# Expert limits searched by base-32 digits of a whole number, and batch folds spread over the items

## The chip, the cores and the metric

The kernel runs on one core of a Trainium2 chip. The metric is the device time of one execution in microseconds (us), the median of several. TensorE (PE in the rows; PEld is its weight load), VectorE (DVE), ScalarE (ACT) and GpSimd (POOL) each run their own list of instructions and wait for each other by semaphores. SyncE (SP) issues most transfers.

## The reference

A two-dimensional Fourier transform (real part) is followed by two mixtures of experts. What the change touches is the transform and the first routing:

```python
X = np.fft.fft(np.fft.fft(x, axis=1), axis=2).real       # x: 4 x 2496 x 256
logits = x @ w_gate                                        # N = 9984 tokens, E = 8 experts
order = np.argsort(-logits.flatten())
for idx in order:                                          # greedy, highest logit first
    tok, e = idx // E, idx % E
    if assigned[tok] >= 0 or counts[e] >= cap: continue    # cap = N // E = 1248
    assigned[tok] = e; counts[e] += 1
...
h = np.maximum(x[mask] @ w1[e], 0.0); out[mask] = h @ w2[e]
# then a second mixture, by argmax, with gates
```

## The kernel before

**First stage: the transform along the sequence.** The list `work_list` has 18 items (batch, part, half). TensorE runs 20 matmuls for an item into two banks; ScalarE copies one bank out (`half`), VectorE joins it with the other (`joined(n)`, two or three instructions of lines 1201 to 1212, which also bump `s_seq`). TensorE may start item n when `joined(n - 3)` is done. Items 0 to 3 are batch 0, items 4 to 7 batch 1, items 8 to 11 batch 2, items 12 and 13 the middle column of all batches, items 14 to 17 batch 3. The input of each batch comes in two transfers and is first folded: `fold(n)` on VectorE (lines 1182 and 1185) makes `even`, a pair on GpSimd (lines 553 and 559) makes `odd`, and ScalarE's `edges(n)` picks two columns. Folds 0 and 1 are batch 0, folds 2 and 3 batch 1, and so on. The table `FOLDS_AT` says after which item's join VectorE issues which fold, and ScalarE the matching `edges`.

**Second stage: features.** 40 tiles, two matmuls each; VectorE copies the odd ones out, ScalarE the even ones, SP stores them.

**Third stage: the search for limits.** Seven phases (`ph`), each closing one expert. In a phase, `name8` finds each token's best open expert (`best`, a one-hot `hot8`), 78 columns of 128 tokens. Then four rounds of `search`: VectorE compares each token's `best` with 32 probes (`above`, four pieces by `CHUNKS`), TensorE counts them per expert with 78 small matmuls whose weights are `above[:, j, :]` (`above_count`), VectorE sets `passes`, one matmul turns them into a step, and VectorE moves the lower bound (`floor`, `move`) and makes the next 32 probes. After the fourth round it marks the tokens above the limit (`new_b`, `ind8`), TensorE counts them (`new_count`, line 819) and then runs `gate_rows` (line 799, 32 matmuls for later use) while VectorE updates the counts and names again. So in each phase but the first, round 0's matmuls stand behind `gate_rows` in TensorE's queue.

**After it** come the slots (one-hot matmuls, from about 369 us) and the two mixtures, from about 412 us to the end.

Of the kernel before, what the change touches and what calls it, by code (L numbers as in the profile page):

```python
# [18 lines left out]
F32 = mybir.dt.float32  # L19
F32R = mybir.dt.float32r  # L20
BF16 = mybir.dt.bfloat16
I32 = mybir.dt.int32
# [6 lines left out]
P = 128  # L29
B, S, D = 4, 2496, 256  # L30
N = B * S
# [23 lines left out]
HOTS = 4  # L55
PROBES = 32
ROUNDS = 4
CHUNKS = (0, 24, 48, 68, N // P)
DCH = D // P
FCH = F // P  # L60

# [17 lines left out]
def turns(gi):  # L79
# [8 lines left out]
_W = [("feat_c", XC), ("feat_s", XC), ("featT_c", 2 * P), ("featT_s", 2 * P), ("ident", P), ("tri", P),  # L88
      ("iota", P), ("prefer", E), ("base1", E), ("base2", E),
      ("sign", 1), ("lane", 1), ("lane2", 1), ("valid", TPE), ("beyond", TPE), ("span", G2 + 1),  # L90
      ("part_lane", NT1), ("fresh4", E * (1 + GT)), ("fresh2", E * 3), ("parts", PROBES * ROUNDS)]
COL = {}
_at = 0
for _n, _w in _W:
# [5 lines left out]
def constants():  # L100

    n = 2 * np.arange(NC * P)[None, :] + np.arange(2)[:, None]
    ang = 2 * np.pi * ((n[:, :, None] * np.arange(KH)) % S) / S
    keep = (n <= HALF)[:, :, None]
    edge = np.where((n == 0) | (n == HALF), 0.5, 1.0)[:, :, None]
    lay = lambda t: np.ascontiguousarray(
        t.reshape(2, NC, P, KH).transpose(2, 0, 1, 3)).astype(np.float32)
    cos_n, sin_n = lay(np.cos(ang) * keep * edge), lay(np.sin(ang) * keep)
    c = np.zeros((P, NCONST), np.float32)

    def put(name, v):
        a, b = COL[name]
        c[:, a:b] = v

    d = np.arange(P)[:, None]
    l = np.arange(XC)[None, :]
    put("feat_c", np.cos(2 * np.pi * ((d * l) % D) / D))
    fs = -np.sin(2 * np.pi * ((d * l) % D) / D)
    fs[0] = (-1.0) ** np.arange(XC)
    put("feat_s", fs)  # L120
    put("featT_c", np.concatenate([c[:, slice(*COL["feat_c"])][:, h * P:(h + 1) * P].T for h in range(2)], 1))
    put("featT_s", np.concatenate([c[:, slice(*COL["feat_s"])][:, h * P:(h + 1) * P].T for h in range(2)], 1))
    put("ident", np.eye(P))
    put("tri", np.arange(P)[:, None] < np.arange(P)[None, :])
    put("iota", np.arange(P)[None, :])
    put("prefer", (E - np.arange(E))[None, :])
    put("base1", (np.arange(E) * TPE * P)[None, :])
    put("base2", (np.arange(E) * REG)[None, :])
    put("span", (np.arange(G2 + 1) * W2)[None, :])
    put("fresh4", (np.arange(E * (1 + GT)) % (1 + GT) != 0)[None, :])  # L130
    put("fresh2", (np.arange(E * 3) % 3 != 0)[None, :])
    p = np.arange(P)[:, None]
    put("sign", np.where(np.arange(P) == 0, 1.0, -1.0)[:, None])
    put("lane", p)
    parts = (np.arange(PROBES) + 1) * float(PROBES) ** -(np.arange(ROUNDS)[:, None] + 1)
    put("parts", parts.reshape(1, -1))
    put("lane2", p + P)
    put("part_lane", p / (np.arange(NT1) + 1.0)[None, :])
    put("valid", (np.arange(TPE) * P + p < CAP))
    put("beyond", 16.0 * E * REG * (np.arange(TPE) * P + p >= CAP))  # L140
    return cos_n, sin_n, c


class Count:
# [5 lines left out]
    def link(self, ins):  # L150

        ins.then_inc(self.sem, 1)
        self.n = self.n + 1
        self.eng.wait_ge(self.sem, self.n)


def build_program(nc, x, x_rev, cos_n, sin_n, const, wg1, w1a, w2a, w2a_t, wg2, wo2, w1b, w2b, out):
    ctx = ExitStack()
    with ctx, nc.allow_non_contiguous_dma("a few rows of logits"):
        def sb(name, shape, dt=F32):  # L160
            return ctx.enter_context(nc.sbuf_tensor(name, shape, dt))
# [88 lines left out]
        def cc(name):  # L250
            return cst[:, COL[name][0]:COL[name][1]]
# [18 lines left out]
        ones_f = sb("ones_f", [1, P])  # L270
        taken = sb("taken", [P, T1])
        first_b = sb("first_b", [P, T1], BF16)
        floor, width = (sb(n, [P, 1]) for n in ("floor", "width"))
        at = 4 * WS + WE + 2 * FCH * GT * P


        def small(w):
            nonlocal at
            at += w
            return arena[:, at - w:at]  # L280

        steps = small(PROBES * ROUNDS)
        probe0 = small(PROBES)
        probe = [small(PROBES) for _ in range(2)]
        at = 4 * WS + WE
        open_log = small(E * NT1).rearrange("p (j e) -> p j e", e=E)
        slow_log = small(E * NT1)
        above = small(NT1 * PROBES // 2).bitcast(BF16).rearrange("p (j k) -> p j k", k=PROBES)
        hot8, ind8 = (small(NT1 * E // 2).bitcast(BF16).rearrange("p (j e) -> p j e", e=E) for _ in range(2))
        hot_b, ind = (small(W8 // 2).bitcast(BF16) for _ in range(2))  # L290
        assert at <= s0
        step_b = sb("step_b", [P, ROUNDS, P], BF16)
        passes = sb("passes", [PROBES, E], BF16)
        new_b = sb("new_b", [P, T1], BF16)
        floors = [sb(f"floor{u}", [P, 1]) for u in range(2)]
        move, top_i = sb("move", [P, 1]), sb("top_i", [P, 1], I32)
        surs = sb("surs", [P, E])
        gone = sb("gone", [P, T1])
# [108 lines left out]
        work_list = [(b, q, h) for b in range(3) for q in range(2) for h in range(2)]  # L407
        work_list += [(0, 2, h) for h in range(2)] + [(3, q, h) for q in range(2) for h in range(2)]
        MID_DONE = 4 * 3 + 2
        FOLDS_AT = {1: (2, 3), 2: (4,), 3: (5,), 4: (6,), 5: (7,)}  # L410
        SEQ_DONE = [4, 8, 12, NU]
        LAST_AT = 5
        assert LAST_AT % 2 and NB % 2
# [303 lines left out]
        def _(pe):  # L717
# [85 lines left out]
            def above_count(n):  # L803

                for c in range(len(CHUNKS) - 1):
                    pe.wait_ge(s_above, n * (len(CHUNKS) - 1) + c + 1)
                    for j in range(CHUNKS[c], CHUNKS[c + 1]):
                        mm = pe.matmul(bank[0][0:PROBES, 0:E], above[:, j, :], hot8[:, j, :],  # L808
                                       start=(j == 0), stop=(j == NT1 - 1))
                mm.then_inc(s_above_ps, 1)  # L810
                pe.wait_ge(s_pass, n + 1)
                pe.matmul(bank[1][:, 0:E], step_b[0:PROBES, n % ROUNDS, :], passes[:], start=True,
                          stop=True).then_inc(s_move_ps, 1)

            def new_count(ph, tokens):
# [332 lines left out]
        def _(dve):  # L1148
# [68 lines left out]
            for n in range(NU):  # L1217
# [5 lines left out]
                if n == NU - 3:  # L1223
                    feature_gates()

            for n in range(1, NB + 1, 2):
                feature_out(dve, dve.tensor_copy, n)

# [20 lines left out]
            dve.memset(zero_u[:], 0)  # L1249
            dve.memset(ones_f[:], 1.0)  # L1250
            dve.memset(ones8[:], 1.0)
            dve.memset(taken[:], FAR)
            dve.memset(gone[:], -FAR)
            dve.memset(left[:], float(CAP))
            dve.memset(first78[:], 1.0)
            link(dve.memset(left_open[:], float(CAP)))
# [1 line left out]
            dve.wait_ge(s_bound_ps, 1)  # L1258
            dve.tensor_reduce(top[0:1, :], bank[1][0:1, 0:P], AX.X, ALU.max).then_inc(s_bound, 1)
            dve.wait_ge(s_bound_ps, 2)  # L1260
            link(dve.tensor_copy(floor[:], bank[1][:, 0:1]))
            link(dve.tensor_scalar(top_i[:], floor[:].bitcast(I32), 0x7F800000, None, ALU.bitwise_and))
            dve.tensor_scalar(width[:], top_i[:].bitcast(F32), 4.0, None, ALU.mult)
            link(dve.tensor_scalar(floor[:], top_i[:].bitcast(F32), -2.0, None, ALU.mult))
            link(dve.tensor_scalar(steps, cc("parts"), width[:], None, ALU.mult))
            link(dve.tensor_scalar(probe0, steps[:, 0:PROBES], floor[:], None, ALU.add))
            for r in range(ROUNDS):
                ins = dve.tensor_scalar(step_b[:, r, :], ones_b[:], width[:], float(PROBES) ** -(r + 1), ALU.mult, ALU.mult)
            link(ins)

            def name8(src):

                link(dve.tensor_reduce(best[:, 0:NT1], src, AX.X, ALU.max))
                link(dve.tensor_tensor(best[:, 0:NT1], best[:, 0:NT1], taken[:, 0:NT1], ALU.min))
                link(dve.tensor_tensor(hot8[:], src, each_e(best), ALU.is_equal))

            def search(ph, r):

                n = ph * ROUNDS + r
                at_ = probe[r % 2] if r else probe0  # L1280
                low, nxt = (floors[(r + u) % 2][:] if r + u else floor[:] for u in range(2))
                for j0, j1 in zip(CHUNKS, CHUNKS[1:]):
                    dve.tensor_tensor(above[:, j0:j1, :], best[:, j0:j1, None].to_broadcast([P, j1 - j0, PROBES]),  # L1283
                                      at_[:, None, :].to_broadcast([P, j1 - j0, PROBES]), ALU.is_ge).then_inc(s_above, 1)
                dve.wait_ge(s_above_ps, n + 1)
                dve.tensor_tensor(passes[:], bank[0][0:PROBES, 0:E], left_open[0:PROBES, :], ALU.is_ge).then_inc(s_pass, 1)
                dve.wait_ge(s_move_ps, n + 1)
                link(dve.tensor_reduce(move[:], bank[1][:, 0:E], AX.X, ALU.max))
                if r + 1 < ROUNDS:
                    dve.tensor_scalar(probe[(r + 1) % 2], steps[:, (r + 1) * PROBES:(r + 2) * PROBES], move[:], low,  # L1290
                                      ALU.add, ALU.add)
                link(dve.tensor_tensor(nxt, low, move[:], ALU.add))

            src = log8
            for ph in range(E - 1):
                name8(src)
                for r in range(ROUNDS):
                    search(ph, r)
                thr_v = floors[ROUNDS % 2][:]
                link(dve.tensor_scalar(new_b[:, 0:NT1], best[:, 0:NT1], thr_v, None, ALU.is_ge))  # L1300
                dve.wait_ge(s_given, ph + 1)
                dve.tensor_tensor(ind8[:], hot8[:], each_e(new_b), ALU.mult).then_inc(s_new, 1)  # L1302
                link(dve.copy_predicated(taken[:, 0:NT1], new_b[:, 0:NT1].bitcast(U16), gone[:, 0:NT1]))
# [437 lines left out]
```

## Time and profile before

| | |
|---|---|
| median of 3 runs | 1447.54 us (1446.55 to 1448.35) |
| profiled execution | 1448.4 us, span 1446.6 us |
| mean granted TensorE clock over the span | 0.899 |
| PE busy | 1291.4 us, 89% |
| DVE busy | 702.1 us, 49% |
| POOL busy | 551.7 us, 38% |
| ACT busy | 336.5 us, 23% |

The span is what lies between the first and the last instruction; the execution's own time has 1.8 us around it. The busy share is an average over stages with different limits, so the stages have to be read one by one.

### The profile page before, as it was taken

Reading aid. Unit: us, or ns where it says so; the run is one execution under the profiler, and the core shown is the slowest. Engines: PE = TensorE matmul, PEld = TensorE weight load, DVE = VectorE, ACT = ScalarE, POOL = GpSimd, SP = SyncE. Lnnn points to the kernel's source line nnn. Section 1 sums busy time; section 2 is a strip of 40 time slices with the busy share of each in tenths; the row PEclk is TensorE's granted clock in tenths of the full one; section 3 lists DMA queues with packets and bytes.
Section 4 is the critical chain, followed back from the end, with each engine's and each line's share of the span. In section 5 each row is a group of like instructions: output and inputs, shape, how many; then the busy total and the mean of one; then the engine's idle time right before and its main releaser. Section 6 shows DMA issues by size and latency. Waiting matters only on the chain.

```text
span 1446.6 us, 31150 instructions
## 1 busy us (share of the span) xinstructions
PE 1291.4 (89%) x10763; PEld 1194.7 (83%) x10764; DVE 702.1 (49%) x1991; ACT 336.5 (23%) x840; POOL 551.7 (38%) x556
## 2 busy tenths in 40 slices
PE   5899657666389999999999999699999999999996
PEld 4567557665179998999989998699999999999996
DVE  2723677776744445444554344634343443343332
ACT  0102100000523333333333233112222222222221
POOL 2800230000035656566564754331344142444411
PEclk9999755555579999999999999799999999999998
DMA  9604620101012221232222222131122222222110
GB/s 346 213 1 152 221 89 31 60 31 60 1 34 92 79 79 62 78 98 77 74 66 79 82 71 77 39 103 44 37 100 73 73 69 73 70 81 95 45 40 23
DMA packets 70726, 116.21 MB, mean 80 GB/s; under 512 B 7784, under 2 KB 50545, under 8 KB 70640
## 3 DMA queue, kind: packets, MB, share of 16 engines
q1 hardware_dynamic: 46864, 72.40, 14.9%
q0 software_dynamic: 11808, 31.03, 6.5%
q10 hardware_dynamic: 11968, 11.63, 2.9%
q8 instruction: 55, 0.90, 0.3%
q14 instruction: 31, 0.25, 0.1%
HBM read 81.87 MB, written 34.45 MB: 80 GB/s over the span
## 4 chain that ended last, share of the span: by engine, by line
PE 75%; DVE 8%; issue 2%; POOL 1%; ACT 1%; DMA 1%; POOLq 0%; DVEq 0%; ACTq 0%
PE bank L869 22%; PE bank L871 22%; PE bank L870 21%; DVE arena L1283 3%; PE bank L799 3%; PE bank L808 3%; PE bank L863 1%; PE bank L950 1%; ACT hot_q L1036 1%; POOL weights_low L575 1%; PE bank L849 1%; DVE hot_r L1448 1%; DVE arena L1290 0%; DVE hot_q L1449 0%; DVE arena L1302 0%
## 5 line engine op out<-in xcount | busy, mean ns | idle before, releaser
L869 PE MATMUL bank<-weights_high,hT_high 128*128 (+1 forms) x1328 | 387.1, 292 | 2.5 <-DVE hT_low L1676 2.5
L870 PE MATMUL bank<-weights_low,hT_high 128*128 (+1 forms) x1328 | 379.3, 286 | 0.0
L871 PE MATMUL bank<-weights_high,hT_low 128*128 (+1 forms) x1328 | 379.2, 286 | 0.0
L869 PE MATMUL bank<-xT_high,weights_high 128*128 128x256 f32 (+1 forms) x1072 | 334.6, 312 | 2.3 <-DVE xT_low L1664 1.3
L871 PE MATMUL bank<-xT_high,weights_low 128*128 128x256 f32 (+1 forms) x1072 | 332.0, 310 | 0.0
L870 PE MATMUL bank<-xT_low,weights_high 128*128 128x256 f32 (+1 forms) x1072 | 331.1, 309 | 0.0
L869 PEld LDWEIGHTS bank<-weights_high,hT_high 128*128 128x128 f32 x1328 | 251.2, 189 | 2.8 <-issue 2.8
L871 PEld LDWEIGHTS bank<-weights_high,hT_low 128*128 128x128 f32 x1328 | 251.5, 189 | 0.0
L870 PEld LDWEIGHTS bank<-weights_low,hT_high 128*128 128x128 f32 x1328 | 250.8, 189 | 0.0
L869 PEld LDWEIGHTS bank<-xT_high,weights_high 128*128 128x128 f32 x1072 | 204.4, 191 | 16.8 <-DVE hT_low L1495 3.2
L871 PEld LDWEIGHTS bank<-xT_high,weights_low 128*128 128x128 f32 x1072 | 203.3, 190 | 11.3
L870 PEld LDWEIGHTS bank<-xT_low,weights_high 128*128 128x128 f32 x1072 | 203.4, 190 | 10.0
L1495 DVE SCALAR_TENSOR_TENSOR hT_low<-bank,hT_high 128x512 fp32r<-128x512 f32 (+1 forms) x192 | 114.4, 599 | 174.9 <-ACT hT_high L1055 168.8
L680 POOL DMA_INDIRECT out_y<-arena,tokb x86 | 84.9, 987 | 289.1 <-DVE tokb L1691 277.0
L1117 ACT ACTIVATE hT_high<-bank 128x512 fp32r<-128x512 f32 x172 | 103.0, 599 | 384.1 <-PE bank L871 384.1
L1676 DVE SCALAR_TENSOR_TENSOR hT_low<-bank,hT_high 128x512 fp32r<-128x512 f32 x172 | 118.4, 691 | 149.4 <-ACT hT_high L1117 141.0
L621 POOL DMA_INDIRECT arena<-spectrum,idxe x80 | 78.5, 982 | 168.7 <-PE bank L863 154.5
L1055 ACT ACTIVATE hT_high<-bank 128x512 fp32r<-128x512 f32 (+1 forms) x192 | 101.4, 528 | 125.5 <-PE bank L871 124.7
L752 PE MATMUL bank<-arena 128*128 128x312 f32 (+3 forms) x360 | 99.5, 439 | 21.2 <-DMA arena<-in_cos 15.0
L1688 DVE TENSOR_SCALAR arena<-bank,gate_tok 128x256 f32<-128x256 f32 x86 | 41.6, 484 | 157.0 <-PE bank L871 118.1
L808 PE MATMUL bank<-arena 128*32 128x8 bf16 x2184 | 69.1, 168 | 47.0 <-DVE arena L1283 45.3
L752 PEld LDWEIGHTS bank<-arena 128*128 128x128 f32 (+1 forms) x360 | 66.0, 185 | 53.3 <-issue 31.0
(232 smaller groups left out, 1446.7 us busy)
## 6 DMA issues: line engine op xcount, KB each, us to landing
arena<-middle ACTq DMA_DIRECT2D x44, 258.0 KB
spectrum<-arena SPq DMA_DIRECT2D x39, 256.0 KB, 2.2
arena<-in_w2a_t SPq DMA_DIRECT2D x8, 1024.0 KB, 5.1
raw<-in_w1a SPq DMA_DIRECT2D x8, 1024.0 KB
raw<-in_w2a SPq DMA_DIRECT2D x8, 1024.0 KB
raw<-in_w1b SPq DMA_DIRECT2D x8, 1024.0 KB
raw<-in_w2b SPq DMA_DIRECT2D x8, 1024.0 KB
arena<-in_x SPq DMA_DIRECT2D x4, 768.0 KB, 4.9
```

The source lines that it names most:

```text
L621: pool.indirect_dma_start(xg4[u], None, spectrum, bass.IndirectOffsetOnAxis(idxe[s][:, k:k + 1], 0)).then_inc(m1.got[u], 16)
L680: pool.indirect_dma_start(out, bass.IndirectOffsetOnAxis(tokb[j][:], 0), yb[j], None, bounds_check=N - 1, oob_is_err=False).then_inc(m2.se ...
L752: mm = pe.matmul(bank[2 * (n % 3) + r][0:m, 0:w], a, t[:, r, c, k0:k1], start=(c == 0), stop=(c == NC - 1))
L799: mm = pe.matmul(bank[3][:, f * LG:(f + 1) * LG], w2_t[:, c, f * P:(f + 1) * P], wgate2[:, c, :], start=(c == 0), stop=(c == DCH - 1))
L808: mm = pe.matmul(bank[0][0:PROBES, 0:E], above[:, j, :], hot8[:, j, :], start=(j == 0), stop=(j == NT1 - 1))
L869: pe.matmul(out_, a[0], b[0], start=start, stop=False)
L870: pe.matmul(out_, a[0], b[1], start=False, stop=False)
L871: return pe.matmul(out_, a[1], b[0], start=False, stop=stop)
L1055: act.activation(hT_split[0][:, f, 0:w], bank[2 + (gi * FCH + f) % 3][:, 0:w], ACT.Relu).then_inc(m1.h_high, 1)
L1117: act.activation(hT_split[0][:, q * FCH // HB:(q + 1) * FCH // HB, 0:W2], bank[H_BANKS[q]][:].rearrange("p (f n) -> p f n", n=W2), ACT.Rel ...
L1495: dve.scalar_tensor_tensor(out=hT_split[1][:, f, 0:w], in0=bank[2 + (gi * FCH + f) % 3][:, 0:w], scalar=0.0, in1=hT_split[0][:, f, 0:w].bi ...
L1676: dve.scalar_tensor_tensor(out=lo, in0=bank[H_BANKS[q]][:].rearrange("p (f n) -> p f n", n=W2), scalar=0.0, in1=hi.bitcast(F32), op0=ALU.m ...
```

## The change

Two edits. First, `FOLDS_AT` spreads folds 4 to 7 over items 3, 5, 7 and 9, where they stood after items 2, 3, 4 and 5. Second, the search works on whole numbers. `best` is scaled and rounded once a phase to a number of 20 bits (`digits[-1]`); the digits by shifts, four of 5 bits each; before each round one instruction subtracts the bound found so far and writes the result as bf16 (`key`). The 32 probes are always 1 to 32, stored once as a bf16 table `probes` of 32 x 78, made by one copy between the first two stages. The compare has the probe as its outer dimension and the column as its inner one, so TensorE's weights are now `above[:, :, j]`: 32 elements, 78 elements (156 bytes) apart, where they were 32 neighbours. Three pieces (12, 28 and 38 columns) stand where there were four (24, 24, 20 and 10).

```diff
-CHUNKS = (0, 24, 48, 68, N // P)
+CHUNKS = (0, 12, 40, N // P)
+BITS = PROBES.bit_length() - 1
+SHIFTS = [BITS * (ROUNDS - 1 - r) for r in range(ROUNDS)]
+LEVELS = 1 << BITS * ROUNDS
...
-        FOLDS_AT = {1: (2, 3), 2: (4,), 3: (5,), 4: (6,), 5: (7,)}
+        FOLDS_AT = {1: (2, 3), 3: (4,), 5: (5,), 7: (6,), 9: (7,)}
...
-                        mm = pe.matmul(bank[0][0:PROBES, 0:E], above[:, j, :], hot8[:, j, :],
+                        mm = pe.matmul(bank[0][0:PROBES, 0:E], above[:, :, j], hot8[:, j, :],
...
+            dve.wait_ge(s_seq, NU)
+            dve.wait_ge(s_half, NU)
+            dve.tensor_copy(probes, iota_b[:, 1:1 + PROBES, None].to_broadcast([P, PROBES, N // P]))
             for n in range(1, NB + 1, 2):
                 feature_out(dve, dve.tensor_copy, n)
...
-            for r in range(ROUNDS):
-                ins = dve.tensor_scalar(step_b[:, r, :], ones_b[:], width[:], float(PROBES) ** -(r + 1), ALU.mult, ALU.mult)
...
                 link(dve.tensor_reduce(best[:, 0:NT1], src, AX.X, ALU.max))
-                link(dve.tensor_tensor(best[:, 0:NT1], best[:, 0:NT1], taken[:, 0:NT1], ALU.min))
-                link(dve.tensor_tensor(hot8[:], src, each_e(best), ALU.is_equal))
+                dve.tensor_tensor(hot8[:], src, each_e(best), ALU.is_equal)
+
+            def whole():
+                link(dve.tensor_scalar(scaled, best[:, 0:NT1], scale[:].bitcast(F32), -0.5 * LEVELS, ALU.mult, ALU.max))
+                link(dve.scalar_tensor_tensor(out=digits[-1], in0=scaled, scalar=0.5 * LEVELS, in1=taken[:, 0:NT1],
+                                              op0=ALU.add, op1=ALU.min))
...
                 for j0, j1 in zip(CHUNKS, CHUNKS[1:]):
-                    dve.tensor_tensor(above[:, j0:j1, :], best[:, j0:j1, None].to_broadcast([P, j1 - j0, PROBES]),
-                                      at_[:, None, :].to_broadcast([P, j1 - j0, PROBES]), ALU.is_ge).then_inc(s_above, 1)
+                    dve.tensor_tensor(above[:, :, j0:j1], key[r % 2][:, None, j0:j1].to_broadcast([P, PROBES, j1 - j0]),
+                                      probes[:, :, j0:j1], ALU.is_ge).then_inc(s_above, 1)
+                if r == 0:
+                    for later in range(1, ROUNDS - 1):
+                        digit(later)
...
                 if r + 1 < ROUNDS:
-                    dve.tensor_scalar(probe[(r + 1) % 2], steps[:, (r + 1) * PROBES:(r + 2) * PROBES], move[:], low,
-                                      ALU.add, ALU.add)
-                link(dve.tensor_tensor(nxt, low, move[:], ALU.add))
+                    link(dve.tensor_scalar(key[(r + 1) % 2], digits[r + 1], move[:], low[r][:], ALU.subtract, ALU.subtract))
+                    dve.tensor_scalar(low[r + 1][:], low[r][:], move[:], float(PROBES) if r + 2 < ROUNDS else 1.0,
+                                      ALU.add, ALU.mult)
```

VectorE's order in the first stage, before, from the end of item 1's join on (lines 1182 and 1185 are a fold, 1201 with 1207 or 1210 a join):

```order
L1185 TENSOR_TENSOR arena<-arena 128x2x2x127
L1201 TENSOR_TENSOR arena<-arena,bank 128x313
L1207 SCALAR_TENSOR_TENSOR arena<-arena,bank 128x312
L1182 TENSOR_TENSOR arena<-arena 128x1536
L1185 TENSOR_TENSOR arena<-arena 128x2x3x127
L1201 TENSOR_TENSOR arena<-arena,bank 128x312
L1207 SCALAR_TENSOR_TENSOR arena<-arena,bank 128x311
L1182 TENSOR_TENSOR arena<-arena 128x1024
```

These are the end of fold 3, join 2, fold 4, join 3 and the start of fold 5. After, at the same place (the lines have moved by four):

```order
L1189 TENSOR_TENSOR arena<-arena 128x2x2x127
L1205 TENSOR_TENSOR arena<-arena,bank 128x313
L1211 SCALAR_TENSOR_TENSOR arena<-arena,bank 128x312
L1205 TENSOR_TENSOR arena<-arena,bank 128x312
L1211 SCALAR_TENSOR_TENSOR arena<-arena,bank 128x311
L1186 TENSOR_TENSOR arena<-arena 128x1536
L1189 TENSOR_TENSOR arena<-arena 128x2x3x127
L1205 TENSOR_TENSOR arena<-arena,bank 128x313
```

Join 3 now stands ahead of fold 4, and join 4 behind it. VectorE's order in the third stage, after, from the naming to round 1 of a phase:

```order
L1278 TENSOR_REDUCE best<-logits 128x78 [waits s_dve]
L1279 TENSOR_TENSOR arena<-logits,best 128x624 [waits s_dve]
L1283 TENSOR_SCALAR arena<-best,scale 128x78
L1284 SCALAR_TENSOR_TENSOR arena<-arena,taken 128x78 [waits s_dve]
L1289 TENSOR_SCALAR arena<-arena 128x78 [waits s_dve]
L1314 CAST arena<-arena 128x78 [waits s_dve]
L1295 TENSOR_TENSOR arena<-arena 128x32x12 [waits s_dve]
L1295 TENSOR_TENSOR arena<-arena 128x32x28
L1295 TENSOR_TENSOR arena<-arena 128x32x38
L1289 TENSOR_SCALAR arena<-arena 128x78 x2
L1301 TENSOR_TENSOR passes<-bank,left_open 32x8 [waits s_above_ps]
```

Lines 1283 to 1314 are four small instructions in a row ahead of the compares, where one small one (line 1274 of before) was.

## Rows read from the trace of the kernel before

**Rows 1.** The page: granted TensorE clock in 40 slices of the span.
```profile
PEclk9999755555579999999999999799999999999998
```
**Rows 2.** Windows by stage; columns: stretch, length, busy us of each engine, clock, DMA.
```profile
0.00:121.40 121.40, 100.23 (x369) 67.13 (x371) 46.52 (x65) 10.66 (x36) 42.46 (x23) 0.97 0.48 167
158.60:355.00 196.40, 126.92 (x2531) 118.80 (x2531) 154.43 (x344) 1.60 (x6) 32.50 (x25) 0.51 0.19 65
```
**Rows 3.** Timeline of TensorE, first stage: start, us, what, idle before.
```profile
54.67 44.74 PE L752 MATMUL bank<-arena 128*128 128x313 f32 x160 [6.20 <-DVE arena L1207]
```
**Rows 4.** Timeline of VectorE, first stage.
```profile
47.90 1.76 DVE L1182 TENSOR_TENSOR arena<-arena 128x1536 f32<-128x1536 f32 x1 [9.93 <-DMA arena<-in_x_rev]
49.70 4.05 DVE L1185 TENSOR_TENSOR arena<-arena 128x762 f32<-128x762 f32 x1
53.67 0.47 DVE L1201 TENSOR_TENSOR arena<-arena,bank 128x312 f32<-128x312 f32 x1
...
54.45 2.04 DVE L1182 TENSOR_TENSOR arena<-arena 128x1024 f32<-128x1024 f32 x1
56.52 2.71 DVE L1185 TENSOR_TENSOR arena<-arena 128x508 f32<-128x508 f32 x1
```
**Rows 5.** Timeline of ScalarE: the copy half way through item 8.
```profile
70.42 0.42 ACT L1018 COPY arena<-bank 128x313 f32<-128x313 f32 x1 [0.64 <-PE bank L752]
```
**Rows 6.** Windows as in rows 2: right after TensorE's stall; then its matmuls alone.
```profile
54.70:59.40 4.70, 4.70 (x9) 3.13 (x10) 4.67 (x3) 0.62 (x3) 4.45 (x3) 0.50 0.86 320
...
60.00:90.00 30.00, 30.00 (x115) 20.82 (x114) 1.00 0.33 114
```
**Rows 7.** Timeline of both engines, a last round of phase 4.
```profile
290.30 0.17 DVE L1288 TENSOR_REDUCE move<-bank 128x1 f32<-128x8 f32 x1 [0.28 <-PE bank L812]
290.90 2.96 DVE L1283 TENSOR_TENSOR arena<-best,arena 128x768 bf16<-128x768 f32 x4
291.91 2.57 PE L808 MATMUL bank<-arena 128*32 128x8 bf16 x78 [1.65 <-DVE arena L1283]
294.52 0.15 DVE L1286 TENSOR_TENSOR passes<-bank,left_open 32x8 bf16<-32x8 f32 x1 [0.65 <-PE bank L808]
295.15 0.16 DVE L1292 TENSOR_TENSOR floor<-floor,move 128x1 f32<-128x1 f32 x1
295.35 0.26 DVE L1300 TENSOR_SCALAR new_b<-best,floor 128x78 bf16<-128x78 f32 x1
```
**Rows 8.** Timeline of both engines, round 0 of phase 5.
```profile
297.04 6.99 PE L799 MATMUL bank<-wgate,arena 128*128 128x16 f32 x32
301.90 2.97 DVE L1283 TENSOR_TENSOR arena<-best,arena 128x768 bf16<-128x768 f32 x4
303.96 2.24 PE L808 MATMUL bank<-arena 128*32 128x8 bf16 x78
306.24 0.15 DVE L1286 TENSOR_TENSOR passes<-bank,left_open 32x8 bf16<-32x8 f32 x1 [1.37 <-PE bank L808]
```
**Rows 9.** VectorE's groups by form, 200 to 345 us: count, busy us, mean ns.
```profile
L1283 DVE TENSOR_TENSOR arena<-best,arena 128x768 bf16<-128x768 f32 x47 | 43.0, 954 | 0.8
L1283 DVE TENSOR_TENSOR arena<-best,arena 128x320 bf16<-128x320 f32 x24 | 11.6, 485 | 0.0
L1302 DVE TENSOR_TENSOR arena<-arena,new_b 128x624 bf16<-128x624 bf16 x5 | 4.0, 809 | 0.2
```
**Rows 10.** The same, 355 to 405 us.
```profile
L1328 DVE TENSOR_TENSOR arena<-arena 128x624 f32<-128x624 f32 x1 | 1.3, 1262 | 1.2 <-issue 1.2
...
L1432 DVE TENSOR_TENSOR arena<-arena 128x624 f32<-128x624 f32 x1 | 0.8, 808 | 0.0
...
L1434 DVE TENSOR_SCALAR pos_i<-pos 128x78 int32<-128x78 f32 x1 | 0.2, 202 | 0.0
```
**Rows 11.** Timeline of VectorE, rounds 2 and 3 of phase 0, beside GpSimd's weight splits.
```profile
176.22 5.92 DVE L1283 TENSOR_TENSOR arena<-best,arena 128x768 bf16<-128x768 f32 x4
...
182.67 0.15 DVE L1286 TENSOR_TENSOR passes<-bank,left_open 32x8 bf16<-32x8 f32 x1 [0.52 <-PE bank L808]
```

More of the change, by code:

```diff
@@ L90 @@
       ("sign", 1), ("lane", 1), ("lane2", 1), ("valid", TPE), ("beyond", TPE), ("span", G2 + 1),
-      ("part_lane", NT1), ("fresh4", E * (1 + GT)), ("fresh2", E * 3), ("parts", PROBES * ROUNDS)]
+      ("part_lane", NT1), ("fresh4", E * (1 + GT)), ("fresh2", E * 3)]
 COL = {}
@@ L134, in constants @@
     put("lane", p)
-    parts = (np.arange(PROBES) + 1) * float(PROBES) ** -(np.arange(ROUNDS)[:, None] + 1)
-    put("parts", parts.reshape(1, -1))
     put("lane2", p + P)
@@ L272, in build_program @@
         first_b = sb("first_b", [P, T1], BF16)
-        floor, width = (sb(n, [P, 1]) for n in ("floor", "width"))
+        bound, scale = sb("bound", [P, 1]), sb("scale", [P, 1], I32)
         at = 4 * WS + WE + 2 * FCH * GT * P
@@ L280, in small @@
             return arena[:, at - w:at]
-        steps = small(PROBES * ROUNDS)
-        probe0 = small(PROBES)
-        probe = [small(PROBES) for _ in range(2)]
+        digits = [small(NT1).bitcast(I32) for _ in range(ROUNDS)]
+        scaled = small(NT1)
+        key = [small(NT1 // 2).bitcast(BF16) for _ in range(2)]
         at = 4 * WS + WE
@@ L287, in build_program @@
         slow_log = small(E * NT1)
-        above = small(NT1 * PROBES // 2).bitcast(BF16).rearrange("p (j k) -> p j k", k=PROBES)
+        above = small(NT1 * PROBES // 2).bitcast(BF16).rearrange("p (k j) -> p k j", k=PROBES)
         hot8, ind8 = (small(NT1 * E // 2).bitcast(BF16).rearrange("p (j e) -> p j e", e=E) for _ in range(2))
@@ L291, in build_program @@
         assert at <= s0
-        step_b = sb("step_b", [P, ROUNDS, P], BF16)
+        at = gates_at + E * FCH * LG
+        probes = small(NT1 * PROBES // 2).bitcast(BF16).rearrange("p (k j) -> p k j", k=PROBES)
+        assert at <= arena_words
+        step_b = sb("step_b", [PROBES, 2, P], BF16)
         passes = sb("passes", [PROBES, E], BF16)
         new_b = sb("new_b", [P, T1], BF16)
-        floors = [sb(f"floor{u}", [P, 1]) for u in range(2)]
+        low = [sb(f"low{u}", [P, 1]) for u in range(ROUNDS)]
         move, top_i = sb("move", [P, 1]), sb("top_i", [P, 1], I32)
@@ L811, in above_count @@
                 pe.wait_ge(s_pass, n + 1)
-                pe.matmul(bank[1][:, 0:E], step_b[0:PROBES, n % ROUNDS, :], passes[:], start=True,
+                pe.matmul(bank[1][:, 0:E], step_b[:, n % ROUNDS == ROUNDS - 1, :], passes[:], start=True,
                           stop=True).then_inc(s_move_ps, 1)
@@ L1251, in _ @@
             dve.memset(ones8[:], 1.0)
-            dve.memset(taken[:], FAR)
-            dve.memset(gone[:], -FAR)
+            dve.memset(taken[:], float(2 * LEVELS))
+            dve.memset(gone[:], -1.0)
+            dve.memset(low[0][:], 0.0)
+            for u, v in enumerate((PROBES, 1)):
+                dve.memset(step_b[:, u, :], float(v))
             dve.memset(left[:], float(CAP))
@@ L1260, in _ @@
             dve.wait_ge(s_bound_ps, 2)
[L1261 to L1266, printed above, removed]
@@ L1267, in _ @@
-            for r in range(ROUNDS):
-                ins = dve.tensor_scalar(step_b[:, r, :], ones_b[:], width[:], float(PROBES) ** -(r + 1), ALU.mult, ALU.mult)
-            link(ins)
+            link(dve.tensor_copy(bound[:], bank[1][:, 0:1]))
+            link(dve.tensor_scalar(top_i[:], bound[:].bitcast(I32), 0x7F800000, None, ALU.bitwise_and))
+            link(dve.tensor_scalar(top_i[:], top_i[:], float(20 << 23), None, ALU.max))
+            link(dve.tensor_scalar(scale[:], top_i[:], -1.0, float((2 * 127 + BITS * ROUNDS - 2) << 23), ALU.mult, ALU.add))
@@ L1277, in search, with digit @@
+            def digit(r):
+                return dve.tensor_scalar(digits[r], digits[-1], SHIFTS[r], None, ALU.arith_shift_right)
             def search(ph, r):
                 n = ph * ROUNDS + r
-                at_ = probe[r % 2] if r else probe0
-                low, nxt = (floors[(r + u) % 2][:] if r + u else floor[:] for u in range(2))
                 for j0, j1 in zip(CHUNKS, CHUNKS[1:]):
-                    dve.tensor_tensor(above[:, j0:j1, :], best[:, j0:j1, None].to_broadcast([P, j1 - j0, PROBES]),
-                                      at_[:, None, :].to_broadcast([P, j1 - j0, PROBES]), ALU.is_ge).then_inc(s_above, 1)
+                    dve.tensor_tensor(above[:, :, j0:j1], key[r % 2][:, None, j0:j1].to_broadcast([P, PROBES, j1 - j0]),
[3 more added lines that the diff above has]
+                        digit(later)
@@ L1296, in _ @@
                 name8(src)
+                whole()
+                link(digit(0))
+                link(dve.tensor_copy(key[0], digits[0]))
                 for r in range(ROUNDS):
                     search(ph, r)
-                thr_v = floors[ROUNDS % 2][:]
-                link(dve.tensor_scalar(new_b[:, 0:NT1], best[:, 0:NT1], thr_v, None, ALU.is_ge))
+                link(dve.tensor_scalar(new_b[:, 0:NT1], digits[-1], move[:], low[-1][:], ALU.subtract, ALU.is_ge))
                 dve.wait_ge(s_given, ph + 1)
```

## The prediction

> **What bounds the kernel now.** I read the page first, then windows by stage, then the timelines of the two stages that the change touches. The page's clock line shows the end of the first stage's worst place (a 6 in slice 2) and a long stretch at the lower of TensorE's two levels, 1.2 GHz [rows 1]. The windows say who waits: until 121.4 us TensorE is busy 100.2 us of it, so that stage is TensorE's, less a wait at the start and one in the middle; from 158.6 to 355 us neither engine is full (PE 126.9, DVE 154.4 of 196.4 us), so the search is a chain that passes between them [rows 2]. The rest of the span is not touched.
>
> In the first stage TensorE sits idle for 6.20 us up to 54.67, released by a join [rows 3]. VectorE's timeline names the cause: fold 4 stands ahead of join 3 in VectorE's queue, waits 9.93 us for its transfer, starts at 47.90 and then takes 1.76 + 4.05 us, so join 3 comes at 53.67 [rows 4]. Behind the idle time the clock stood at 0.50 for 4.7 us, with 9 matmuls started in it [rows 6]; at the full level 115 start in 30 us, 0.261 us each, so 9 more would have fitted.
>
> In the search a plain round goes: `move` at 290.30, compares at 290.90, first matmul at 291.91 (1.01 later), `passes` at 294.52, 3.62 after the compares began. The 78 matmuls take as long as the four compares do, shifted by one piece [rows 7]. Round 0 of a phase is different: the compares begin at 301.90 but TensorE is in `gate_rows` until 303.96, and `passes` follows 2.28 us after that [rows 8]. This is the price of 78 matmuls with everything ready: 28.7 ns each (2.24 / 78).
>
> **Edit 1, the folds.** Nothing is added, four folds move. Join 3 no longer waits for fold 4: item 3's matmuls are over at about 38.3 (item 5's end at 48.47, from rows 3, less two items of 5.1 to 5.2), so item 6 can start at 48.47 without a wait. What is late next: fold 4 still starts at 47.90, since its transfer lands then, and still meets GpSimd; join 4 comes behind it at 53.7 and ends at 54.5, so item 7 starts at 54.6 where item 6 ended at 53.7: 0.9 us idle. Join 5 and fold 5 follow (0.9 + 2.0 + 2.7 us [rows 4]), to 60.1, and item 8 needs fold 5: it starts at 60.1, 0.3 us late. Fold 6 (to 67.8) and fold 7 (to about 75.5) stand ahead of joins 8 and 10, which items 11 and 13 want at 75.9 and later, so nothing waits for them. Before, ScalarE's copy half way through item 8 began at 70.42 [rows 5], ten matmuls of 0.261 us behind its start at 67.8. So item 8 comes 67.8 - 60.1 = **7.7 us** earlier, and items 8 to 17 run as before. If the 0.9 us gap costs clock as the old one did, 9 matmuls of 0.261, or 2.4 us, come off, and 5.3 stay. I take 7.7: the old drop came after 6.20 us of idling, the new gaps are 0.9 and 0.3. ScalarE's `edges` move with the folds, the loads of x are released by folds that end before GpSimd's do, and GpSimd's queue is unchanged: nothing for these.
>
> **The stored table** is one copy of 2496 elements behind the last join. At one element in 1.05 ns (below) it takes 2.6 us, with two at a time 1.3. The features stage has four banks, so TensorE wants VectorE's first tile only at its sixth, over 4 us on: I cost it at nothing; without that cover it would be 1.3 to 2.6 us.
>
> **Edit 2, one round.** The compares of before run one element per cycle: 954 ns for 768 and 485 ns for 320 [rows 9], 1.05 ns an element and some 150 ns fixed, of which back to back only about 60 show. No two-input bf16 instruction at twice that rate stands in the trace; the only one of that kind, line 1302, takes 809 ns for 624 bf16 elements [rows 9], the slow rate, but reads an operand that repeats each element. So both ends: 1.04 or 0.52 ns an element. I take 0.52, since now all three operands are bf16 with neighbours in the inner dimension, which neither row has. The Trainium skill ("VectorE: DVE Perf Modes", section "The perf-mode tier table") gives a `tensor_tensor` in bf16 twice the fp32 rate, and the microarchitecture page ("Vector Engine (DVE) Microarchitecture Reference", section 5.1) says that a row read again and again keeps it and an element read again and again does not, with which line 1302 agrees.
>
> Pieces of 384, 896 and 1216 elements then reach TensorE at 0.42, 0.95 and 1.64 us after the first begins (0.20, 0.47 and 0.63 us of streaming, 0.06 between two, 0.22 for the signal, which is 1.01 less 768 elements' 0.80). Twelve matmuls end at 0.77, the next 28 run from 0.95 to 1.75, the last 38 to 2.84: `passes` at 2.88, where it was at 3.62. TensorE binds now. Ahead of the compares, `key` (78 columns, as line 1300: 0.29 to the next) and `low` (0.08, which nothing waits for) replace probes and `floor`: 0.57 us where 0.60 were. So **0.77 us a round**. In round 0 of phases 1 to 6 four small instructions (0.20 to 0.24 us each, line 1434 [rows 10]) stand where one of about that length was, and `hot8` is not waited for: the compares begin 0.65 us later, at 302.55 on rows 8's scale, the last piece is ready at 304.2, and TensorE, free at 303.96, wants it at 305.1. `gate_rows` hides it all: nothing, and without that cover +0.65.
>
> The sum: 18 plain rounds of 0.77, 13.9. The mark needs no `floor` first (295.15 to 295.35 [rows 7]): 7 x 0.19 = 1.3. Phase 0: rounds 0 and 1, 1.5; rounds 2 and 3 run beside GpSimd's splits, where the compares take 5.92 us and `passes` comes 6.45 after their start [rows 11], twice the 2.96 alone: with the wait kept at about 0.74 a piece (2.96 / 4) three pieces make 1.5 + 2.2, then 0.2 + 1.1 for TensorE, 5.1: 2.6 for both; set-up 0.3. **19.6 us** in all, and with edit 1 **27.3**. The profiled execution took 1448.4, 0.9 above the median of 1447.54; 1447.5 less 27.3 is **1420**.
>
> **Rivals.** (a) *The weights are read slowly.* Each of the 78 matmuls of a round now loads 32 elements that lie 156 bytes apart. The trace has no such load. Its nearest rows of spread reads are VectorE's: line 1328 reads a bf16 operand at steps of 16 bytes and takes 1262 ns for 624, line 1432 without steps 808 [rows 10]: 0.73 ns more for each. From below the price is nothing (a load of neighbours hides in 28.7 ns). From above, 32 x 0.73 = 23 ns a matmul, 52 in place of 28.7. I take nothing, because the row that shares the instruction is TensorE's own, and it asks for an element only every 0.9 ns (28.7 / 32); but this is the weakest step. At 23 ns a round's TensorE time grows by 1.8: round 0 of six phases +10.8, plain rounds -0.77 + 1.8 - 0.2 (it no longer waits for piece two) = +0.85, 15.3 over 18; phase 0 about -0.5, marks -1.3, folds -7.7: +16.6, **1464**. Each ns more adds 28 x 0.078 = 2.2 us. It decides above 27.3 / 2.2 = 12.5 ns a matmul. This is the case on the other side. The Trainium skill speaks for it ("SBUF — State Buffer", note on cachelines): an access that goes to a new 16-byte line each time pays, bf16 steps up to 8 elements are free, and here the step is 78. By that rule the time is this rival's.
>
> (b) *The compares stay at one element per cycle.* Then pieces are ready at 0.62, 1.61 and 2.94, and 38 matmuls behind the last, not 10, end at 4.07: +0.42 a round, 7.6 over 18, +0.4 for six rounds 0, about 1 in phase 0, less 1.6 and 7.7: **1449**, no change to be told.
>
> (c) *The folds give back less*: item 7's gap costs clock, or GpSimd's pair and the folds meet longer. Then 5.3 or less of the 7.7: **1423**. For it: GpSimd is full in that stretch. Against it: the fold that meets it is the same.
>
> **How the numbers follow.** The forecast with its own spread (1414 to 1427, (c) in it) has 0.52; a small price for the weights, below the deciding one, 0.08 (1427 to 1445); (b) 0.07; (a) 0.33. The rows alone would split (a) evenly with the forecast; I go lower as TensorE asks for an element only each 0.9 ns. A measurement tells 0.2%, 2.9 us, from no change. Faster: 0.52 + 0.08 + a little of (b), 0.61; same 0.06; slower 0.33. The range reaches from 1414 to 1473, which leaves out some 0.1 of (a) above and a little below; the likeliest case's own is 1414 to 1427.
>
> **What would show it.** PE's timeline: 160 or more matmuls in a row around 48 us with gaps under 1.5 us in sum, and the first stage ending near 113.8 in place of 121.5. Compare forms 128x1216 near 0.75 us by mean (right) or near 1.4 (b). A run of 78 matmuls behind `gate_rows` in 2.2 us (right) or 3.5 to 4.5 (a). A plain round of 3.9 us from `move` to `move`, where it was 4.65. The limits, were they not found exactly in 20 bits, would send the kernel into its exact search of 32 rounds a phase, hundreds of us; the step of the whole numbers is that of before (4 x the largest power of two over 2^20), so I give it nothing. The prediction is wrong if the weights cost over 12.5 ns, or if TensorE's clock falls for longer once the stages move.

## The result, and the profile after

The changed kernel took 1487.54 us (median of 4 runs, 1486.24 to 1487.86), the kernel before 1447.94 us beside it (4 runs, 1446.55 to 1448.78): a ratio of 1.0273, 95% interval 1.0255 to 1.0291. It is slower by 39.6 us, where 1420 was predicted and 1414 to 1473 was the range.

First the stage of the first edit. The timeline of TensorE in the changed kernel (start, us, what, idle before), which answers to [rows 3]:

```profile
15.04 76.64 PE L756 MATMUL bank<-arena 128*128 128x313 f32 x280 [15.04 <-DMA arena<-in_cos]
91.61 1.06 PE L730 MATMUL bank<-wgate,cst 128*128 128x8 f32 x8
92.53 21.29 PE L756 MATMUL bank<-arena 128*128 128x313 f32 x80
113.66 0.62 PE L777 MATMUL bank<-feat_c,arena 128*128 128x273 f32 x2
```

The 6.20 us of waiting in [rows 3] are gone, all 280 matmuls of items 0 to 13 stand in one piece, and the features begin at 113.66. In the kernel before they began 7.7 us later, at 121.38:

```profile
121.38 0.62 PE L773 MATMUL bank<-feat_c,arena 128*128 128x273 f32 x2
```

This edit gave the time that was predicted, to a tenth.

Then the search. The timeline of both engines in a last round of the changed kernel, which answers to [rows 7]:

```profile
279.94 0.17 DVE L1303 TENSOR_REDUCE move<-bank 128x1 f32<-128x8 f32 x1 [0.28 <-PE bank L816]
280.14 0.32 DVE L1305 TENSOR_SCALAR arena<-arena,move,low 128x78 bf16<-128x78 int32 x1
280.50 0.21 DVE L1306 TENSOR_SCALAR low<-low,move 128x1 f32<-128x1 f32 x1
280.63 1.58 DVE L1295 TENSOR_TENSOR arena<-arena 128x384 bf16<-128x384 bf16 x3
...
281.03 4.81 PE L812 MATMUL bank<-arena 128*32 128x8 bf16 x78 [1.13 <-DVE arena L1295]
285.88 0.15 DVE L1301 TENSOR_TENSOR passes<-bank,left_open 32x8 bf16<-32x8 f32 x1 [3.67 <-PE bank L812]
...
286.32 0.17 DVE L1303 TENSOR_REDUCE move<-bank 128x1 f32<-128x8 f32 x1 [0.28 <-PE bank L816]
286.52 0.32 DVE L1317 TENSOR_SCALAR new_b<-arena,move,low 128x78 bf16<-128x78 int32 x1
286.87 0.81 DVE L1319 TENSOR_TENSOR arena<-arena,new_b 128x624 bf16<-128x624 bf16 x1
```

The compares shrank from 2.96 us to 1.58, and the first matmul follows them after 0.40 us, not 1.01. But the 78 matmuls now take 4.81 us by themselves, and VectorE sits idle for 3.67 us before `passes`. The round from one `move` to the next (279.94 to 286.32) is 6.38 us, where it was 4.65. Round 0 of the next phase, which answers to [rows 8], shows the matmuls with hardly a compare beside them:

```profile
288.26 6.99 PE L803 MATMUL bank<-wgate,arena 128*128 128x16 f32 x32
...
293.78 1.59 DVE L1295 TENSOR_TENSOR arena<-arena 128x384 bf16<-128x384 bf16 x3
...
295.18 4.82 PE L812 MATMUL bank<-arena 128*32 128x8 bf16 x78
...
300.04 0.15 DVE L1301 TENSOR_TENSOR passes<-bank,left_open 32x8 bf16<-32x8 f32 x1 [4.45 <-PE bank L812]
```

The last piece ended at 295.37, 0.2 us after the matmuls began at 295.18 and long before its turn, and still 78 matmuls take 4.82 us, where [rows 8] has 2.24: 61.8 ns each, not 28.7. The groups by form, 190 to 370 us of the changed kernel (count, busy us, mean ns):

```profile
L812 PE MATMUL bank<-arena 128*32 128x8 bf16 x1669 | 103.1, 201 | 18.1 <-DVE arena L1295 18.1
L812 PEld LDWEIGHTS bank<-arena 128*32 128x32 bf16 x1670 | 101.3, 155 | 19.7 <-DVE arena L1295 19.5
...
L1295 DVE TENSOR_TENSOR arena<-arena 128x1216 bf16<-128x1216 bf16 x22 | 17.2, 784 | 0.0
...
L1295 DVE TENSOR_TENSOR arena<-arena 128x384 bf16<-128x384 bf16 x22 | 7.7, 351 | 0.2
```

The same two groups of the kernel before, 200 to 345 us:

```profile
L808 PE MATMUL bank<-arena 128*32 128x8 bf16 x1847 | 57.8, 168 | 31.0 <-DVE arena L1283 29.7
L808 PEld LDWEIGHTS bank<-arena 128*32 128x32 bf16 x1848 | 53.7, 103 | 34.7 <-DVE arena L1283 34.1
```

The weight load takes 155 ns where it took 103, and the matmul's own record 201 where it had 168. Both grew, the load by more, and only the load's operand changed its layout: `hot8[:, j, :]`, which the matmul streams, lies as before. Loads and matmuls of neighbours overlap, so neither duration is the price; that is the growth from 28.7 to 61.8 ns. The compares run at (784 - 351) / 832 = 0.52 ns an element, twice the rate of [rows 9].

The bookkeeping closes: 18 plain rounds of +1.73 are 31.1 us, six rounds 0 of +2.58 (4.86 after `gate_rows` in place of 2.28) are 15.5, six marks of -0.14 are -0.8, set-up and phase 0 are +1.7 (from the end of the features to the second naming it is 38.78 us, where it was 37.04), the folds are -7.7: 39.8 of the measured 39.6.

### The profile page after: what moved, and what is told of

Same layout as the page of the kernel before. It is cut to its first block, busy times and chain, and to the rows that moved or that the text cites. A ratio compares the mean times of both kernels' runs of the same rounds, so it can differ in the third digit from the quotient of the medians.

```text
span 1486.1 us, 31148 instructions
## 1 busy us (share of the span) xinstructions
PE 1355.7 (91%) x10763; PEld 1262.5 (85%) x10764; DVE 665.7 (45%) x1988; ACT 335.7 (23%) x840; POOL 546.9 (37%) x556
## 4 chain that ended last, share of the span: by engine, by line
PE 79%; DVE 5%; issue 2%; POOL 1%; ACT 1%; DMA 1%; POOLq 0%; DVEq 0%; ACTq 0%
PE bank L873 21%; PE bank L875 21%; PE bank L874 21%; PE bank L812 9%; PE bank L803 3%; PE bank L867 1%; PE bank L954 1%; ACT hot_q L1040 1%; DVE arena L1295 1%; POOL weights_low L579 1%; DVE arena L1305 1%; PE bank L853 1%; DVE hot_r L1465 0%; DVE hot_q L1466 0%; DVE arena L1319 0%
## 5 line engine op out<-in xcount | busy, mean ns | idle before, releaser
L812 PE MATMUL bank<-arena 128*32 128x8 bf16 x2184 | 135.2, 201 | 30.5 <-DVE arena L1295 30.5
L812 PEld LDWEIGHTS bank<-arena 128*32 128x32 bf16 x2184 | 132.5, 155 | 32.8 <-DVE arena L1295 32.6
```

Of the source, the lines that this page charges most:

```text
L812: mm = pe.matmul(bank[0][0:PROBES, 0:E], above[:, :, j], hot8[:, j, :], start=(j == 0), stop=(j == NT1 - 1))
```

## The experiments

Theory A: the distance between a matmul's 32 weights costs TensorE time. Rival B: something else in the new compares does (their bf16 writes beside TensorE's reads, the new pieces). From here on, "ns a matmul" is the length of a run of 78 over 78. It holds some 0.15 us that a run has once: with neighbours 38 take 1.17 us and 78 take 2.24, so one more adds 26.8 ns. The differences between layouts are not touched by it.

**Only the layout turned.** The kernel before, with the compares written probe by probe:

```diff
-above = ...rearrange("p (j k) -> p j k", k=PROBES)
+above = ...rearrange("p (k j) -> p k j", k=PROBES)
-  mm = pe.matmul(bank[0][0:PROBES, 0:E], above[:, j, :], hot8[:, j, :],
+  mm = pe.matmul(bank[0][0:PROBES, 0:E], above[:, :, j], hot8[:, j, :],
+  dve.tensor_tensor(above[:, :, j0:j1], best[:, None, j0:j1].to_broadcast([P, PROBES, j1 - j0]),
+                    at_[:, :, None].to_broadcast([P, PROBES, j1 - j0]), ALU.is_ge)
```

> The kernel before with one thing of the change: the compares write probe by probe, column by column, so that a matmul's 32 weights lie 156 bytes apart. Compares stay fp32, four pieces, folds as before. Theory A (the distance of the weights costs): 78 matmuls in 4.8 us in every round, in place of 2.24 to 2.57; a plain round grows by about 2.3 us, round 0 behind gate_rows by 2.6, in all some 28 x 2.3 = 60 us, about 1510 us. Rival B (the new bf16 compares or their instructions slow TensorE's reads, not the distance): matmuls stay at 2.24 to 2.57 us, the time stays near 1448.

Measured: 1506.7 us (one run; before 1447.4). Its timeline of TensorE, with fp32 compares:

```profile
274.78 4.82 PE L808 MATMUL bank<-arena 128*32 128x8 bf16 x78
```

The same 4.82 us as in the changed kernel, with the old fp32 compares and the old four pieces: the layout is enough, and B is not needed.

**Only the layout kept.** The changed kernel with the probe innermost, so the key repeats each element:

```diff
+above = ...rearrange("p (j k) -> p j k", k=PROBES)
+  mm = pe.matmul(bank[0][0:PROBES, 0:E], above[:, j, :], hot8[:, j, :],
+  dve.tensor_tensor(above[:, j0:j1, :], key[r % 2][:, j0:j1, None].to_broadcast([P, j1 - j0, PROBES]),
+                    iota_b[:, None, 1:1 + PROBES].to_broadcast([P, j1 - j0, PROBES]), ALU.is_ge)
```

> The changed kernel, but with the probe innermost, so that a matmul's 32 weights are neighbours again; the compare then reads a key that repeats each element. Theory A: matmuls at 28.7 ns, 2.24 us for 78; compares at one element per 1.04 ns, pieces of 384, 896, 1216 elements, so passes comes about 4.07 us after the compares begin, and the time is 1447.5 - 7.7 (folds) + about 9 = 1447 to 1450. Rival B: matmuls stay near 62 ns, and the time stays at 1487 or rises.

Measured: 1454.5 us (one run). Its timeline, one round:

```profile
258.17 0.17 DVE L1303 TENSOR_REDUCE move<-bank 128x1 f32<-128x8 f32 x1 [0.28 <-PE bank L816]
258.37 0.32 DVE L1305 TENSOR_SCALAR arena<-arena,move,low 128x78 bf16<-128x78 int32 x1
258.73 0.21 DVE L1306 TENSOR_SCALAR low<-low,move 128x1 f32<-128x1 f32 x1
258.86 2.89 DVE L1295 TENSOR_TENSOR arena<-arena,iota_b 128x384 bf16<-128x384 bf16 x3
...
261.80 1.17 PE L812 MATMUL bank<-arena 128*32 128x8 bf16 x38 [0.43 <-DVE arena L1295]
263.01 0.15 DVE L1301 TENSOR_TENSOR passes<-bank,left_open 32x8 bf16<-32x8 f32 x1 [1.26 <-PE bank L812]
```

38 matmuls take 1.17 us, the packed price, with the new bf16 compares and the new pieces beside them: B is out as a part of the cause too. The time missed the expected 1447 to 1450 by 4.5 us, most of which is in the 18 plain rounds: `passes` comes at 4.15 after the compares begin (4.07 expected), and from `move` to the compares it is 0.69 us (258.17 to 258.86), not 0.57, since `low` waits for `key` and takes 0.21. All three operands are bf16 here, and still the compares run at (1418 - 551) / 832 = 1.04 ns an element, where the changed kernel has 0.52. Like line 1302 of [rows 9], they read one element again and again, so that is the likely reason. This run also starts `iota_b` at its second element, and no run takes the two apart.

**Weights 2 elements apart.** Columns in groups of JB, so that the inner rows of the compares are JB long and the weights JB apart:

```diff
+above = ...rearrange("p (g k j) -> p g k j", k=PROBES, j=JB)
+  mm = pe.matmul(bank[0][0:PROBES, 0:E], above[:, j // JB, :, j % JB], hot8[:, j, :],
+  dve.tensor_tensor(above[:, g0:g1],
+      key[r % 2][:, j0:j1].rearrange("p (g j) -> p g j", j=JB)[:, :, None, :].to_broadcast([P, g1 - g0, PROBES, JB]),
+      probes[:, None, :, :].to_broadcast([P, g1 - g0, PROBES, JB]), ALU.is_ge)
```

> The changed kernel with the columns in groups of 2: group, probe, column within the group. A matmul's 32 weights are then 2 elements (4 bytes) apart. 80 columns are compared in pieces of 16, 32, 32 (two of padding), the stored table shrinks to 64 elements. Theory A in the form of lines of 16 bytes: a load at 4 bytes costs as one of neighbours, 28.7 ns a matmul. If the compares keep two elements a cycle with rows of 2, passes comes 2.9 us after the compares begin and the time is about 1420; if they fall to one a cycle, 3.9 us and about 1447. Rival C (any distance but 1 element costs): matmuls at 62 ns, about 1488.

Measured: 1425.26 us (4 runs, 1424.79 to 1425.59), ratio to before 0.9845 (0.9828 to 0.9861). The timeline of TensorE:

```profile
260.73 2.24 PE L814 MATMUL bank<-arena 128*32 128x8 bf16 x78
...
264.60 2.42 PE L814 MATMUL bank<-arena 128*32 128x8 bf16 x78 [1.20 <-DVE arena L1300]
```

2.24 us for 78 behind `gate_rows`, as in [rows 8]: weights 4 bytes apart are free. The compares keep the double rate with rows of two (685 ns for 1024 elements, 418 for 512). Rival C is out. The time is 5 above the expected 1420: the longer step from `move` to the compares seen above, 0.12 us a round, is 2.2 of it over 18 rounds, and the rest is not accounted for.

**The price by distance.** Groups of 80, 4, 8 and 16 columns, with the pieces and the padding of the run with 2:

> The changed kernel with rows of 80 columns in place of 78, pieces of 16, 32, 32: weights 160 bytes apart, a multiple of 16 and 32 bytes, with half of the columns still at an odd place in their 4 bytes. Theory A (any far distance costs the same): 62 ns a matmul, about 1488. Rival D (the odd pitch of 156 bytes is what costs, by lines or banks that it straddles): another price, under 50 or over 75 ns a matmul, and the time by 2.2 us for each ns.

> As the run with groups of 2 (1425.3 us), with groups of 4 columns: weights 4 elements, 8 bytes, apart. Theory A with lines of 16 bytes: two weights share a line, a matmul stays at 28.7 to 31 ns, about 1425. Rival E (the unit is 8 bytes): each weight opens a new one, about 60 ns a matmul, about 1488.

> Groups of 8: weights 16 bytes apart. Theory A: every weight in a line of its own, 60 ns or more a matmul, 1485 or more. Rival F (only far distances, over 64 bytes, cost): 28.7 to 31 ns and about 1425.

> Groups of 16: weights 32 bytes apart. Theory A without more: the same price as at 16 bytes. But 160 bytes cost 82 ns and 156 bytes 62 ns a matmul, so the distance matters beyond the line; if even multiples of 16 bytes cost more, 82 ns or above and 1530 or above.

And the changed kernel with its rows set 79, 80 and 128 columns apart:

```diff
-above = small(NT1 * PROBES // 2)....rearrange("p (k j) -> p k j", k=PROBES)
+above = small(80 * PROBES // 2)....rearrange("p (k j) -> p k j", k=PROBES)[:, :, 0:NT1]
```

> The changed kernel with the rows of the compares' result 79 columns apart in place of 78: weights 158 bytes apart, never a multiple of 4. If the price is one opened line for each weight: 62 ns a matmul, 1487 to 1490, as at 156 bytes. If it goes by how many weights meet in the same bank: another price.

> The changed kernel, its own pieces of 12, 28, 38, with rows 80 apart: 160 bytes, as in the run at 1533.5 us but with nothing else changed. If the distance alone made that price: 82 ns a matmul, 78 in 6.4 us, and about 1533. If the pieces or the padding did: 62 ns and 1488.

> Rows 128 apart: 256 bytes. If distances that are multiples of 16 bytes are as slow as 160 bytes once they are far: 82 ns and 1533. If it goes by a power of two in the distance (banks): over 100 ns, over 1570. If 160 bytes is an exception: 62 ns, 1488.

Measured, each one run, with the run of 78 matmuls behind `gate_rows` (or, at 80, the plain one, which is the same to 0.01):

| bytes apart | ns a matmul | over 28.7 | us |
|---|---|---|---|
| 4 | 28.7 | 0 | 1425.3 |
| 8 | 35.4 | 6.7 | 1435.2 |
| 16 | 62.1 | 33.4 | 1490.2 |
| 32 | 63.7 | 35.0 | 1492.7 |
| 156 (the change) | 61.8 | 33.1 | 1487.5 |
| 158 | 73.3 | 44.6 | 1512.9 |
| 160, groups of 80 | 82.1 | 53.4 | 1533.5 |
| 160, rows of 80 | 82.1 | 53.4 | 1532.9 |
| 256 | 58.8 | 30.1 | 1479.3 |

The rows of seven of them, TensorE's timelines at 8, 16, 32 and 158 bytes, 160 with groups and with rows of 80, and 256 bytes, in that order, a fence each:

```profile
265.05 2.76 PE L814 MATMUL bank<-arena 128*32 128x8 bf16 x78
```
```profile
262.98 4.84 PE L814 MATMUL bank<-arena 128*32 128x8 bf16 x78
```
```profile
263.24 4.97 PE L814 MATMUL bank<-arena 128*32 128x8 bf16 x78
```
```profile
272.01 5.72 PE L812 MATMUL bank<-arena 128*32 128x8 bf16 x78
```
```profile
257.19 6.40 PE L814 MATMUL bank<-arena 128*32 128x8 bf16 x78 [1.20 <-DVE arena L1299]
```
```profile
249.33 6.40 PE L812 MATMUL bank<-arena 128*32 128x8 bf16 x78 [1.14 <-DVE arena L1295]
```
```profile
258.57 4.59 PE L812 MATMUL bank<-arena 128*32 128x8 bf16 x78
```

What follows: at 4 bytes a load is free, at 16 bytes the price is there in full, and rivals E (a unit of 8 bytes) and F (only far distances) are out. At 8 bytes the forecast of theory A, 28.7 to 31 ns and 1425 us, missed as well: 35.4 ns, a fifth of the full price, and 10 us of the time. The compares take the same 684 or 685 and 418 ns at 4, 8, 16 and 32 bytes, so VectorE's work is the same in these runs. The load's own duration goes with it (medians 103, 117, 156 and 158 ns at 4, 8, 16 and 32 bytes, 155, 177, 192 and 150 at 156, 158, 160 and 256). Beyond 16 bytes the distance does not order the price: 160 bytes cost most with either set of pieces, 158 lie between it and 156, and 256, which I had thought could be worst, is the cheapest of the far ones. Rival D has half its point: the whole price at 156 bytes is not an accident of that pitch, but pitches differ by up to 23 ns. The expectations of one price for all far distances (62 ns) and of over 100 ns at 256 both missed. By what rule the far pitches differ is open; no run here tells it apart.

**The folds alone.** The kernel before with only the new `FOLDS_AT`:

> The kernel before with the folds of the change alone. By the prediction's first edit the first stage ends 7.7 us earlier, TensorE's 6.20 us of idling and the 4.7 us at the lower clock are gone, and the time is 1447.5 - 7.7 = 1439.8. Rival (something later takes it back): under 3 us.

Measured: 1439.79 us (4 runs, 1439.13 to 1441.2) against 1447.51, ratio 0.9943 (0.9927 to 0.9960): 7.7 us. Its first stage ends at 114.09, 7.3 us earlier than in the trace of before. Nothing takes it back later.

**Both edits, weights 2 apart, four pieces, no padding.**

```diff
-CHUNKS = (0, 16, 48, 80)
+CHUNKS = (0, 8, 24, 46, 78)
```

> The version with groups of 2 (1425.3 us), without padding and with pieces of 8, 16, 22, 32 columns. From rows of that version (0.26 us from a piece's end of streaming to the first matmul, two elements in 1.04 ns, 0.06 between pieces) pieces are ready at 0.35, 0.68, 1.11, 1.70 us and TensorE ends at 2.70, passes at 2.75 in place of 2.93: 0.18 us for 22 rounds, 1421.3. Rival (a fourth instruction and signal costs what the early start gives): 1425.

Measured: 1422.52 us (5 runs, 1421.08 to 1423.31), ratio to before 0.9822 (0.9809 to 0.9836): the fastest version, 25.6 us below the kernel before it (1448.10) and 65 below the changed one. `passes` comes 2.77 us after the compares begin (2.75 expected), the round is 3.89 us, where the run with three pieces has 4.05. The fourth piece gave 2.7 us of the 4.0 forecast:

```profile
266.39 1.66 DVE L1298 TENSOR_TENSOR arena<-arena 128x256 bf16<-128x256 bf16 x4
...
266.73 2.39 PE L814 MATMUL bank<-arena 128*32 128x8 bf16 x78 [1.06 <-DVE arena L1298]
269.16 0.15 DVE L1305 TENSOR_TENSOR passes<-bank,left_open 32x8 bf16<-32x8 f32 x1 [1.11 <-PE bank L814]
```

## Why the prediction was wrong

**Folds.** Right in size and cause: 7.7 predicted, 7.7 measured alone. Of the two gaps that I had put in, the 0.3 us shows nowhere. The 0.9 us before item 7, behind join 4, is in five of the twelve traces with the new table (0.72 to 1.04 us, granted clock 1.00 on both sides of it), as here in the fastest version:

```profile
54.34 37.18 PE L758 MATMUL bank<-arena 128*128 128x312 f32 x140 [0.81 <-DVE lastA L1218]
```

In the other seven, the changed kernel's and the folds' own among them, the first item ended later (its join at 22.6 to 23.6 us, not 22.0 to 22.2), item 6 with it, and join 4 was done in time. So in the changed kernel a slower start of 1.04 us (23.32 against 22.28 before) hid the gap; with it or without, the stage ends at 113.3 to 114.1 in all twelve. That the trace has no gap there is luck, that the sum holds is not. The late item's first weight loads start 0.52 us apart until 20.39 us, where before it was until 18.23, with the granted clock at 1.00 in both; why is open. A small slip beside it: no 6 stands in the clock line of [rows 1]; the 4.7 us at the lower clock show in [rows 6] alone.

**The stored table.** Right: nothing. From the first matmul of the features to the first instruction behind them it is 38.22 us in both kernels (121.38 to 159.60, 113.66 to 151.88).

**The compares.** Right: 0.52 ns an element, first matmul at 0.40 us (0.42). **Round 0's preparation.** Right: from the read of the counts to the compares it is 5.23 us (288.55 to 293.78 in the changed kernel), 4.58 before, 0.65 more, and hidden. **The step from `move` to the compares.** Mis-sized: I had 0.57 us, it is 0.69. From `key` to `low` it is 0.36 where I had 0.29, and from `low` to the compares 0.13 where I had 0.08. That is 0.12 a round, 2.2 us over 18 rounds: small here, and a part of the 2 to 5 us by which the versions with weights 4 bytes apart lie above my sum. **The marks.** Mis-sized: 0.14 us each, not 0.19, since the first instruction behind `move` takes 0.32 in place of 0.26.

**The weights.** This is the step that failed: "From below the price is nothing ... I take nothing". The price is 33.1 ns a matmul, and `passes` comes 5.25 us after the compares begin, not 2.88. It was named as the weakest step and the case behind it was worked out, with its deciding point (12.5 ns) and its mechanism; but I gave it 0.33, and I closed it upward at 23 ns by VectorE's 0.73 ns an element. TensorE's own is 33.1 / 32 = 1.03 ns. With that number the rival's sum gives 1464 + 10.1 x 2.2 = 1486, which is the time measured within 2 us; the 2.2 us of the step above are what it lacks. Two errors of reasoning lie in it. I excused TensorE because it asks for an element every 0.9 ns only, but VectorE asks only every 1.04 ns and pays all the same, so that was no reason at all. And I took a row of another engine as the upper end of a price, where it was only the nearest one.

The Trainium skill ("SBUF — State Buffer", note on cachelines) was right on the case: an access to a new line of 16 bytes each time pays. The trace agrees for a load at 16 bytes or more, 30.1 to 53.4 ns for 32 weights. By that note a bf16 step of up to 8 elements is free; here 4 elements cost 6.7 ns and 8 elements 33.4, so for this load only the step of 2 elements is shown free, and 4 already cost something. How the price differs among the far pitches the note does not say, and the runs leave it open.

## What to carry to other kernels

When a layout is turned so that one engine reads rows, look at who reads the columns: 32 bf16 weights 16 bytes or more apart took TensorE over twice as long as neighbours, more than VectorE won. Both can have their way: an inner group of two elements gives VectorE its double rate and leaves the weights 4 bytes apart. And at every wait of the bounding engine it is worth looking for a queue in which an instruction that waits for a transfer stands ahead of work that is ready: four folds moved, fold 4 behind join 3 above all, gave 7.7 us.

## What was not expected of the hardware

The price of far weights does not grow with distance: 33.1 ns at 156 bytes, 44.6 at 158, 53.4 at 160 (twice, with different pieces), 30.1 at 256. VectorE kept 0.52 ns an element with inner rows of only two elements, (685 - 418) / 512, whose key is read again for each of 32 probes. TensorE was at its lower level (1.2 GHz; granted clock 0.50 from 170 to 320 us in every run) for all these matmuls; what the loads cost at the higher one was not measured.
